# Attention, MoE and gated softmax in one kernel: the 1e-9 of the denominators is summed from memory instead of added

## The chip, the cores and the metric

The kernel runs on one core of a Trainium2 chip. The metric is the device time of one execution in microseconds (us); the kernel before has a median of 773.45 us over three runs. TensorE is called PE (its weight loads PEld), VectorE DVE, ScalarE ACT, GpSimd POOL, and the queue that issues most DMAs SP.

## The reference

Three stages follow each other. Only the first matters here: an attention over keys and values averaged in groups of four rows ("pooled"), plus an attention over the seven keys nearest to each query ("local"). Both softmaxes add 1e-9 to the sum of the exponentials.

```python
def sm_attn(qq, kk, vv):
    s = scale * np.matmul(qq, kk.transpose(0, 1, 3, 2))
    s = s - np.max(s, axis=-1, keepdims=True)
    a = np.exp(s)
    a = a / (np.sum(a, axis=-1, keepdims=True) + 1e-09)
    return np.matmul(a, vv)
# q_d, k_d, v_d: means over factor = 4 rows; batch 4, heads 8, seq 576, head_dim 64
out_d = sm_attn(q_d, k_d, v_d)
out_up = np.repeat(out_d, factor, axis=2)
mask = np.abs(pos[:, None] - pos[None, :]) < factor
# local: scores masked, exp, / (sum + 1e-09), times v
x = out_up + out_local            # to [2304, 512]
x = (x @ w_a) * (x @ w_b) @ w_out # 512 -> 1536 -> 512
# then h = x @ w_in (512 -> 1024), h * softmax(h), layer norm, @ w_out2
```

## The kernel before

The 2304 tokens are handled in six tiles of 384. Every product of the second and third stage is made of three fp32r matmuls (high by high, high by low, low by high; lines 956 to 958), and these fill PE. The attention is done beside them.

**The head.** The first tile's attention runs before the large products. Its pooled part works on four pairs of heads: ACT writes the exponentials of a pair to `p_head` and their sums, by the accumulator of the activation, to `hp_sum` [96, 4, 2] (`head_pooled_exp`, line 1157). DVE makes `hp_den` = (`hp_sum` + 1e-9) * 4 in one tensor_scalar (`head_pooled_norm`, line 1496) and its reciprocal `hp_inv`; the factor 4 is there because `v_d` holds sums of four rows and not means. The turned exponentials are copied from PSUM to `pT_head` by ACT (line 1169). Some matmuls on ones (line 738, `keep_busy`, reading `xup`, which DVE's first instruction fills at line 1688) keep PE occupied.

**Pooled jobs.** Batches 1 to 3 and the rest of batch 0 have their pooled attention in 20 jobs, placed by a hand-written table of (tile, slot) between PE's large products. A job is: scores (PE, line 889), maximum (DVE, 1473), exponential with its sum into `pool_sum` [128, 2] (ACT, 1177), turn (PE, 899), copy to `pT_pool` (ACT, 1186), `pool_den` = (`pool_sum` + 1e-9) * 4 (DVE tensor_scalar, 1479), reciprocal `pool_inv` (DVE, 1482), values (PE, 913), and the output scaled by `pool_inv` (ACT, 1195) and stored.

**Units of the local attention.** For tiles 1 to 5 the local attention is done on DVE, in ten units (two for each tile), each in 18 steps spread over the slots by `local_at`. Seven products q*k and seven reductions (lines 1588 and 1597) give the scores `p_u` [128, 7, 12]. Then come a minimum with the edge mask (1605), the maximum over seven (1606), the subtraction (1607), the exponential on ACT (1215), the sum over seven (1612), the 1e-9 (1613, `u_den`), the reciprocal (1614) and the normalisation (1615). Twenty-odd products with v (1628, 1636, 1642, 1646) and one addition with the pooled part (1652, into `accT`) end the unit. PE turns `accT` (line 924), ACT and DVE split the result into the next tile's `x_hi` (1261) and `x_lo` (1547).

DVE's queue is in program order. Between the steps of the units stand the pooled jobs' steps and those of the large products: `gate` (1554, reads the b product from PSUM), `ab_low` (1558), `wo_low` (1537). POOL runs the low halves of the weights (1900, 1908) and sums of raw rows (1881, 1888) at its own pace, from the point on at which ACT or a DMA has brought their inputs.

Of the kernel before, what the change touches and what calls it, by code (L numbers as in the profile page):

```python
# [5 lines left out]
FP32 = mybir.dt.float32  # L6
FP32R = mybir.dt.float32r
ALU = mybir.AluOpType
ACT = mybir.ActivationFunctionType
# [4 lines left out]
R4 = 4  # L14
# [143 lines left out]
def build_program(nc, q, k, v, w_a, w_b, w_out, w_in, w_out2, g_ln, out):  # L158
# [46 lines left out]
    g_sb = place("g_sb", [128, GC], FP32)  # L205
    p_u = place("p_u", [128, EDGE, HPP * TPP], FP32)
    u_max = place("u_max", [128, HPP * TPP], FP32)
    u_sum = place("u_sum", [128, HPP * TPP], FP32)
    u_den = place("u_den", [128, HPP * TPP], FP32)
    u_inv = place("u_inv", [128, HPP * TPP], FP32)  # L210
    pool_bias = place("pool_bias", [128, 2], FP32)
    pool_sum = place("pool_sum", [128, 2], FP32)
    pool_den = place("pool_den", [128, 2], FP32)
    pool_inv = place("pool_inv", [128, 2, 2], FP32)
    hp_bias = place("hp_bias", [96, PPB, 2], FP32)
    hp_sum = place("hp_sum", [96, PPB, 2], FP32)
    hp_den = place("hp_den", [96, PPB, 2], FP32)
# [141 lines left out]
    with ctx:  # L359
# [757 lines left out]
        def _(act):  # L1117
# [36 lines left out]
            def head_pooled_exp(c):  # L1154
                act.wait_ge(s.hp_bias_ready, c + 1 if c < 2 else PPB)
                for h in range(2):
                    last = A(p_head[:, c, h, :], hp_scores(c, h), ACT.Exp,
                             bias=hp_bias[:, c, h:h + 1], accum_out=hp_sum[:, c, h:h + 1])
                last.then_inc(s.hp_exped, 1)
# [7 lines left out]
            def head_pooled_pT(c):  # L1167
                act.wait_ge(s.hp_turned, c + 1)
                A(pT_head[:, c, :], bank(HP_T[c], 4 * 96, SH), ACT.Copy).then_inc(s.hp_pT_ready, 1)

            def pooled_exp(i):
                at_least(act, s.p_turned, i)
                act.wait_ge(s.pool_bias_ready, i + 1)
                at_least(act, s.pool_inv_ready, i)
                count, _ = job_rows(i)
                for h in range(2):
                    last = A(p_pool[0:count, h, :], bank(XB[h], SD, count), ACT.Exp,
                             bias=pool_bias[0:count, h:h + 1],
                             accum_out=pool_sum[0:count, h:h + 1])
                last.then_inc(s.pool_exped, 1)  # L1180

            def pT_copy(i):
                at_least(act, s.out_mm_d, i)
                act.wait_ge(s.p_turned, i + 1)
                count, _ = job_rows(i)
                A(pT_pool[:, :, 0:count], bank(XB[1])[0:SH].rearrange("p (x e) -> p x e", x=4)[:, :, 0:count], ACT.Copy
                  ).then_inc(s.pT_out, 1)

# [24 lines left out]
            def unit_exp(u):  # L1213
                act.wait_ge(s.u_sub_ready, u - 1)
                A(p_u[:, :, :], p_u[:, :, :], ACT.Exp, scale=SCALE).then_inc(s.u_exped, 1)

# [195 lines left out]
        def _(dve):  # L1412
# [63 lines left out]
            def pooled_inverse(i):  # L1476
                dve.wait_ge(s.pool_exped, i + 1)
                count, _ = job_rows(i)
                chain.link(V.tensor_scalar(pool_den[0:count, :], pool_sum[0:count, :], 1e-9, float(R4),
                                           ALU.add, ALU.mult))  # L1480
                at_least(dve, s.out_d_ready, i - 1)
                V.reciprocal(pool_inv[0:count, i % 2, :], pool_den[0:count, :]).then_inc(s.pool_inv_ready, 1)
# [11 lines left out]
            def head_pooled_norm(c):  # L1494
                dve.wait_ge(s.hp_exped, c + 1)
                chain.link(V.tensor_scalar(hp_den[:, c, :], hp_sum[:, c, :], 1e-9, float(R4), ALU.add, ALU.mult))
                if c >= 2:
# [76 lines left out]
            def local_step(m, g, step, marks, used):  # L1574
# [25 lines left out]
                if step == EDGE + 1:  # L1600
                    local.wait()
                    dve.wait_ge(s.edge_ready, 2)
                    limit = edge[:, m % 3].unsqueeze(2).to_broadcast([128, EDGE, HPP, TPP])
                    by_head = p_u[:, :, :].rearrange("p e (h t) -> p e h t", t=TPP)
                    local.link(V.tensor_tensor(by_head, by_head, limit, ALU.min))
                    local.link(V.tensor_reduce(u_max[:, :], p_u[:, :, :].rearrange("p e n -> p n e"), AX.X, ALU.max))
                    V.tensor_tensor(p_u[:, :, :], p_u[:, :, :],
                                    u_max[:, :].unsqueeze(1).to_broadcast([128, EDGE, HPP * TPP]), ALU.subtract
                                    ).then_inc(s.u_sub_ready, 1)
                if step == EDGE + 2:  # L1610
                    dve.wait_ge(s.u_exped, u - 1)
                    local.link(V.tensor_reduce(u_sum[:, :], p_u[:, :, :].rearrange("p e n -> p n e"), AX.X, ALU.add))
                    local.link(V.tensor_scalar(u_den[:, :], u_sum[:, :], 1e-9, None, ALU.add))
                    local.link(V.reciprocal(u_inv[:, :], u_den[:, :]))
                    V.tensor_tensor(p_u[:, :, :], p_u[:, :, :],
                                    u_inv[:, :].unsqueeze(1).to_broadcast([128, EDGE, HPP * TPP]), ALU.mult
# [70 lines left out]

            V.memset(xup[:, 0:2, :], 1.0).then_inc(s.ones_ready, 1)
            head_qT(0)
            head_kT(0)  # L1690
# [305 lines left out]
```

## Time and profile before

| | us |
|---|---|
| median of 3 runs | 773.45 |
| lowest, highest of the 3 | 771.84, 1066.27 |
| the profiled execution | 773.61 |
| its span in the trace | 771.5 |

| engine | busy us | share of the span |
|---|---|---|
| PE | 759.5 | 98% |
| PEld | 702.9 | 91% |
| DVE | 547.9 | 71% |
| ACT | 301.6 | 39% |
| POOL | 174.6 | 23% |

The three runs agree to about 2 us but for one far above the others. The profiled execution lies 2.1 us above its own span: that much lies around the part which the trace shows. A busy share says how full an engine is over the whole span, and not whether another engine waits for it at a given point: that is read from idle times and what ended them. Times of single instructions are shown in us from the span's start.

### The profile page before, as it was taken

The page shows a single profiled execution, that of the slowest core. Times are in us where ns is not written, and L with a number is a line of the kernel's source. Part 1 is how long each engine was busy: PE and PEld are TensorE (multiplying, and loading weights), DVE is VectorE, ACT ScalarE, POOL GpSimd, SP SyncE. Part 2 cuts the span into 40 slices and gives each one's busy share as a digit, 9 for nine tenths or more (in the row PEclk, how much of TensorE's full clock was granted, in tenths as well). Part 3 has the DMA queues.
Part 4 walks back from the last instruction along what each step waited for, and adds up shares of the span by engine and source line. Part 5 has one row for each costly group of instructions (what it writes and reads, how often), then busy time and mean ns, then how long its engine had stood idle before and what let it go on. Part 6 is the DMA issues. An engine that isn't in the chain of part 4 may idle for free.

```text
span 771.5 us, 12627 instructions
## 1 busy us (share of the span) xinstructions
PE 759.5 (98%) x4616; PEld 702.9 (91%) x4616; DVE 547.9 (71%) x990; ACT 301.6 (39%) x824; POOL 174.6 (23%) x216
## 2 busy tenths in 40 slices
PE   8999999999999999999999999999999999999998
PEld 7889999999999999999999999999988888888886
DVE  5699889989877887797876874023377666666663
ACT  4656446463524434362525343234422222222222
POOL 3349460184444030060001121111100000000000
PEclk9899999999999999999999999999999999999999
DMA  9999947778789575573645523736111111011011
GB/s 179 220 218 228 215 109 219 229 208 237 216 207 257 150 209 153 160 199 114 178 140 165 164 93 103 232 100 202 40 57 56 40 43 55 28 55 55 28 42 41
DMA packets 94650, 108.84 MB, mean 141 GB/s; under 512 B 29309, under 2 KB 62589, under 8 KB 94589
## 3 DMA queue, kind: packets, MB, share of 16 engines
q1 hardware_dynamic: 83293, 99.38, 48.6%
q10 hardware_dynamic: 11296, 8.65, 3.7%
q8 instruction: 37, 0.61, 0.3%
q14 instruction: 24, 0.20, 0.1%
HBM read 87.46 MB, written 20.55 MB: 140 GB/s over the span
## 4 chain that ended last, share of the span: by engine, by line
PE 94%; DVE 2%; SPq 2%; DMA 1%; issue 1%; ACT 0%; DVEq 0%
PE psum L956 28%; PE psum L958 27%; PE psum L957 27%; PE psum L1083 2%; PE psum L913 2%; PE psum L889 1%; PE psum L865 1%; PE psum L924 1%; PE psum L899 1%; DMA v_h<-in_v 1%; SPq L483 1%; SPq L477 1%; SPq L492 1%; PE psum L794 1%; PE psum L738 0%
## 5 line engine op out<-in xcount | busy, mean ns | idle before, releaser
L956 PE MATMUL psum<-x_hi,w_hi 128*128 128x384 f32 x576 | 198.1, 344 | 0.2 <-DVE x_lo L1547 0.2
L958 PE MATMUL psum<-x_hi,w_lo 128*128 128x384 f32 x576 | 193.0, 335 | 0.0
L957 PE MATMUL psum<-x_lo,w_hi 128*128 128x384 f32 x576 | 192.7, 335 | 0.0
L956 PEld LDWEIGHTS psum<-x_hi,w_hi 128*128 128x128 f32 x576 | 108.2, 188 | 3.7 <-issue 2.9
L957 PEld LDWEIGHTS psum<-x_lo,w_hi 128*128 128x128 f32 x576 | 108.3, 188 | 0.0
L958 PEld LDWEIGHTS psum<-x_hi,w_lo 128*128 128x128 f32 x576 | 108.1, 188 | 0.0
L956 PE MATMUL psum<-ab_hi,wo_hi 128*128 128x384 f32 x288 | 99.6, 346 | 0.7 <-DVE wo_lo L1537 0.7
L958 PE MATMUL psum<-ab_hi,wo_lo 128*128 128x384 f32 x288 | 96.5, 335 | 0.0
L957 PE MATMUL psum<-ab_lo,wo_hi 128*128 128x384 f32 x288 | 96.4, 335 | 0.0
L1554 DVE TENSOR_TENSOR ab_f<-psum,a_sb 128x384 f32<-128x384 f32 x72 | 39.9, 554 | 76.9 <-PE psum L958 53.7
L1266 ACT ACTIVATE a_sb<-psum 128x384 f32<-128x384 f32 x72 | 35.3, 490 | 109.9 <-PE psum L958 108.4
L1271 ACT ACTIVATE ab_hi<-ab_f 128x384 fp32r<-128x384 f32 x72 | 37.6, 523 | 93.6 <-DVE ab_f L1554 90.6
L1588 DVE TENSOR_TENSOR tmp<-q_u,k_u 128x768 f32<-128x768 f32 x70 | 71.5, 1025 | 0.0
L1914 POOL TENSOR_TENSOR ab_lo<-ab_f,ab_hi 128x384 fp32r<-128x384 f32 x24 | 28.5, 1188 | 182.7 <-ACT ab_hi L1271 182.7
L1597 DVE TENSOR_REDUCE p_u<-tmp 128x12 f32<-128x768 f32 x70 | 66.0, 942 | 0.1
L1881 POOL TENSOR_TENSOR raw<-raw 96x256 f32<-96x256 f32 x42 | 39.3, 959 | 109.1 <-DMA raw<-in_q 54.6
L1303 ACT ACTIVATE e_sb<-psum,neg_max 128x1024 f32<-128x1024 f32 x18 | 20.1, 1117 | 108.6 <-DVE neg_max L1771 108.6
L956 PE MATMUL psum<-w_hi,lnT_hi 128*128 128x512 f32 x144 | 57.6, 400 | 0.0
L956 PEld LDWEIGHTS psum<-ab_hi,wo_hi 128*128 128x128 f32 x288 | 54.1, 188 | 3.0 <-issue 2.8
L958 PE MATMUL psum<-w_hi,lnT_lo 128*128 128x512 f32 x144 | 56.3, 391 | 0.0
L956 PE MATMUL psum<-win_hi,y_hi 128*128 128x512 f32 x144 | 56.1, 390 | 0.0
L958 PE MATMUL psum<-win_hi,y_lo 128*128 128x512 f32 x144 | 56.1, 389 | 0.0
(163 smaller groups left out, 1364.6 us busy)
## 6 DMA issues: line engine op xcount, KB each, us to landing
wo_hi<-wo_hi_scratch SPq DMA_DIRECT2D x53, 256.0 KB, 2.7
wo_lo<-wo_lo_scratch SPq DMA_DIRECT2D x53, 256.0 KB, 3.0
wo_raw<-in_moe_w_out SPq DMA_DIRECT2D x19, 256.0 KB, 5.6
yT_scratch<-y_sb ACTq DMA_DIRECT2D x6, 768.0 KB, 4.7
y_raw<-yT_scratch SPq DMA_DIRECT2D x18, 256.0 KB, 3.0
out<-out_sb SPq DMA_DIRECT2D x18, 256.0 KB, 2.1
k_u<-in_k SPq DMA_DIRECT2D x11, 384.0 KB
v_u<-in_v SPq DMA_DIRECT2D x11, 384.0 KB
```

What stands on the lines that cost most here:

```text
L913: last = mm(bank(XB[0])[p0:p0 + n, SD + h * D:SD + (h + 1) * D], pT_pool[:, 2 * h + kh, p0:p0 + n], v_d[:, pair, kh, h * D:(h + 1) * D], s ...
L956: mm(dst, wh, xh, start=first, stop=False, skip_group_check=not check)
L957: mm(dst, wh, xl, start=False, stop=False, skip_group_check=not check)
L958: last = mm(dst, wl, xh, start=False, stop=end, skip_group_check=not check)
L1266: A(a_sb[:, g % 2, :], bank(GA, NT), ACT.Copy).then_inc(s.a_copied, 1)
L1271: A(ab_hi[:, g % 2, :], ab_f[:, g % 2, :], ACT.Copy).then_inc(s.ab_hi_ready, 1)
L1303: A(e_sb[:, par, :], psum[:, HB[par][0] * BANK:HB[par][0] * BANK + F2], ACT.Exp, bias=neg_max[:, par:par + 1], accum_out=e_sum[:, par:par ...
L1554: V.tensor_tensor(ab_f[:, g % 2, :], bank(GB, NT), a_sb[:, g % 2, :], ALU.mult).then_inc(s.ab_ready, 1)
L1588: last = V.tensor_tensor(tmp[:, step % 3], q_u[:, :, :], k_u[:, :, step * D:step * D + TPP * D], ALU.mult)
L1597: last = V.tensor_reduce(p_u[:, step - 1, :], tmp[:, (step - 1) % 3] .rearrange("p h (t d) -> p (h t) d", d=D), AX.X, ALU.add)
L1881: last = G.tensor_tensor(t[:, :, i, 0:128], t[:, :, i, 0:128], t[:, :, i, 128:256], ALU.add)
L1914: G.tensor_tensor(ab_lo[:, g % 2, :], ab_f[:, g % 2, :], ab_hi[:, g % 2, :], ALU.subtract).then_inc(s.ab_lo_by_pool, 1)
```

## The change

The constant is no longer added by an instruction. It lies in memory beside the sums, and the sum takes it in:

- `p_u` gets an eighth row, filled with 1e-9 once at the start. The sum of a unit goes over eight rows instead of seven, `u_den` and its instruction are gone, and the reciprocal reads `u_sum`. All other accesses of `p_u` are cut to the first seven rows.
- `pool_sum` and `hp_sum` get a last axis of two. ACT writes the sum to element 0, element 1 holds 1e-9. `pool_den` and `hp_den` are a tensor_reduce over that axis instead of a tensor_scalar.
- The factor 4 that this tensor_scalar also applied goes as 1/4 into the scale of ACT's copies to `pT_head` and `pT_pool`.
- Three memsets on DVE, behind the one of `xup`, write the constants.
- With `u_den` gone and `p_u` larger, what is placed behind them in SBUF (`q_u`, `k_u`, `v_u`, `tmp`, `raw`, `qdT`, `win_hi` and others) lies 64 bytes lower.

```diff
-    p_u = place("p_u", [128, EDGE, HPP * TPP], FP32)
+    p_u = place("p_u", [128, EDGE + 1, HPP * TPP], FP32)
-    u_den = place("u_den", [128, HPP * TPP], FP32)
-    pool_sum = place("pool_sum", [128, 2], FP32)
+    pool_sum = place("pool_sum", [128, 2, 2], FP32)
-    hp_sum = place("hp_sum", [96, PPB, 2], FP32)
+    hp_sum = place("hp_sum", [96, PPB, 2, 2], FP32)
...
-                A(pT_head[:, c, :], bank(HP_T[c], 4 * 96, SH), ACT.Copy).then_inc(s.hp_pT_ready, 1)
+                A(pT_head[:, c, :], bank(HP_T[c], 4 * 96, SH), ACT.Copy, scale=1.0 / R4).then_inc(s.hp_pT_ready, 1)
...
-                             accum_out=pool_sum[0:count, h:h + 1])
+                             accum_out=pool_sum[0:count, h, 0:1])
...
-                A(p_u[:, :, :], p_u[:, :, :], ACT.Exp, scale=SCALE).then_inc(s.u_exped, 1)
+                A(p_u[:, 0:EDGE, :], p_u[:, 0:EDGE, :], ACT.Exp, scale=SCALE).then_inc(s.u_exped, 1)
...
-                chain.link(V.tensor_scalar(pool_den[0:count, :], pool_sum[0:count, :], 1e-9, float(R4),
-                                           ALU.add, ALU.mult))
+                chain.link(V.tensor_reduce(pool_den[0:count, :], pool_sum[0:count, :, :], AX.X, ALU.add))
...
-                chain.link(V.tensor_scalar(hp_den[:, c, :], hp_sum[:, c, :], 1e-9, float(R4), ALU.add, ALU.mult))
+                chain.link(V.tensor_reduce(hp_den[:, c, :], hp_sum[:, c, :, :], AX.X, ALU.add))
...
                     local.link(V.tensor_reduce(u_sum[:, :], p_u[:, :, :].rearrange("p e n -> p n e"), AX.X, ALU.add))
-                    local.link(V.tensor_scalar(u_den[:, :], u_sum[:, :], 1e-9, None, ALU.add))
-                    local.link(V.reciprocal(u_inv[:, :], u_den[:, :]))
-                    V.tensor_tensor(p_u[:, :, :], p_u[:, :, :],
+                    local.link(V.reciprocal(u_inv[:, :], u_sum[:, :]))
+                    V.tensor_tensor(p_u[:, 0:EDGE, :], p_u[:, 0:EDGE, :],
...
             V.memset(xup[:, 0:2, :], 1.0).then_inc(s.ones_ready, 1)
+            V.memset(hp_sum[:, :, :, :], 1e-9)
+            V.memset(pool_sum[:, :, :], 1e-9)
+            V.memset(p_u[:, EDGE, :], 1e-9)
```

No queue is reordered. On DVE, around the third pooled job and the softmax of the second unit (the job's `pool_den` is the first row), the program of before has:

```order
L1479 TENSOR_SCALAR pool_den<-pool_sum 128x2
L1482 RECIPROCAL pool_inv<-pool_den 128x2
L1597 TENSOR_REDUCE p_u<-tmp 128x12
L1537 TENSOR_TENSOR wo_lo<-wo_raw,wo_hi 128x512
L1605 TENSOR_TENSOR p_u<-p_u,edge 128x84
L1606 TENSOR_REDUCE u_max<-p_u 128x12
L1607 TENSOR_TENSOR p_u<-p_u,u_max 128x84
L1612 TENSOR_REDUCE u_sum<-p_u 128x12
L1613 TENSOR_SCALAR u_den<-u_sum 128x12
L1614 RECIPROCAL u_inv<-u_den 128x12
L1615 TENSOR_TENSOR p_u<-p_u,u_inv 128x84
```

The same place in the program of after:

```order
L1478 TENSOR_REDUCE pool_den<-pool_sum 128x2
L1480 RECIPROCAL pool_inv<-pool_den 128x2
L1595 TENSOR_REDUCE p_u<-tmp 128x12
L1535 TENSOR_TENSOR wo_lo<-wo_raw,wo_hi 128x512
L1603 TENSOR_TENSOR p_u<-p_u,edge 128x84
L1604 TENSOR_REDUCE u_max<-p_u 128x12
L1605 TENSOR_TENSOR p_u<-p_u,u_max 128x84
L1610 TENSOR_REDUCE u_sum<-p_u 128x12
L1611 RECIPROCAL u_inv<-u_sum 128x12
L1612 TENSOR_TENSOR p_u<-p_u,u_inv 128x84
```

One row is gone, one has another operation, the order is the same. In all, DVE has ten rows fewer (`u_den`) and three more (the memsets).

## Rows read from the trace of the kernel before

**Rows 1.** The page: busy us (share of the span) xinstructions
```profile
PE 759.5 (98%) x4616; PEld 702.9 (91%) x4616; DVE 547.9 (71%) x990; ACT 301.6 (39%) x824; POOL 174.6 (23%) x216
```

**Rows 2.** Timeline of PE: start us, us, instruction [idle before <-releaser]
```profile
128.48 0.52 PE L924 MATMUL psum<-ident,accT 128*128 128x128 f32 x3 [1.12 <-DVE accT L1652]
...
188.80 0.52 PE L924 MATMUL psum<-ident,accT 128*128 128x128 f32 x3 [0.97 <-DVE accT L1652]
```

**Rows 3.** PE's waits: engine line, waited for: us in total, times, longest
```profile
PE psum L956 <- DVE wo_lo L1537: 0.7, 1, 0.7
PE psum L889 <- DVE x_lo L1547: 0.5, 1, 0.5
```

**Rows 4.** Windows: length; busy us of PE, PEld, DVE, ACT, POOL; clock; DMA, GB/s
```profile
26.00:28.00 2.00, 2.00 (x11) 1.93 (x10) 0.61 (x3) 1.65 (x7) 0.89 (x1) 0.50 1.16 203
99.10:128.40 29.30, 28.25 (x192) 25.80 (x190) 28.53 (x45) 17.30 (x53) 11.85 (x12) 1.00 0.53 148
200.00:771.50 571.50, 567.74 (x3194) 523.20 (x3192) 377.21 (x677) 200.16 (x519) 79.22 (x96) 1.00 0.41 118
```

**Rows 5.** Lines by form: busy us, mean ns of one | idle before, releaser
```profile
L1479 DVE TENSOR_SCALAR pool_den<-pool_sum 96x2 f32<-96x2 f32 x12 | 3.5, 288 | 0.0
L1613 DVE TENSOR_SCALAR u_den<-u_sum 128x12 f32<-128x12 f32 x10 | 2.0, 204 | 0.3
L1150 ACT ACTIVATE qdT<-psum 128x288 f32<-128x288 f32 x6 | 4.1, 760 | 3.3 <-PE psum L865 3.0 <-PE psum L871 0.3
L1150 ACT ACTIVATE kdT<-psum 128x288 f32<-128x288 f32 x6 | 4.0, 740 | 7.4 <-PE psum L865 5.9 <-PE psum L871 0.9 <-ACT y_sb L1276 0.5
```

**Rows 6.** Timeline of DVE, third pooled job and second unit
```profile
109.41 0.70 DVE L1479 TENSOR_SCALAR pool_den<-pool_sum 128x2 f32<-128x2 f32 x1
...
114.01 0.17 DVE L1613 TENSOR_SCALAR u_den<-u_sum 128x12 f32<-128x12 f32 x1
114.22 0.23 DVE L1614 RECIPROCAL u_inv<-u_den 128x12 f32<-128x12 f32 x1
```

**Rows 7.** Single lines of DVE: duration ns min/median/max, first and last start us, forms
```profile
L1479 DVE TENSOR_SCALAR pool_den<-pool_sum x20: 154/158/894, 56.1 to 457.0; 96x2 f32<-96x2 f32 x12, 128x2 f32<-128x2 f32 x8
L1612 DVE TENSOR_REDUCE u_sum<-p_u x10: 286/304/309, 65.9 to 451.3; 128x12 f32<-128x84 f32 x10
L1597 DVE TENSOR_REDUCE p_u<-tmp x70: 934/942/954, 47.7 to 447.5; 128x12 f32<-128x768 f32 x70
L1771 DVE TENSOR_REDUCE neg_max<-part_max x18: 154/155/155, 558.0 to 750.9; 128x1 f32<-128x2 f32 x18
L1615 DVE TENSOR_TENSOR p_u<-p_u,u_inv x10: 245/247/579, 66.9 to 452.1; 128x84 f32<-128x84 f32 x10
```

**Rows 8.** Timeline of POOL, where the first `pool_den` of rows 6 runs
```profile
109.35 0.73 POOL L1900 TENSOR_TENSOR w_lo<-w_raw,w_hi 128x256 fp32r<-128x256 f32 x1 [0.60 <-ACT w_hi L1236]
```

**Rows 9.** Timeline of DVE ahead of the second turn
```profile
156.63 0.31 DVE L1612 TENSOR_REDUCE u_sum<-p_u 128x12 f32<-128x84 f32 x1 [2.71 <-ACT p_u L1215]
...
157.44 0.58 DVE L1615 TENSOR_TENSOR p_u<-p_u,u_inv 128x84 f32<-128x84 f32 x1
...
175.20 2.74 DVE L1588 TENSOR_TENSOR tmp<-q_u,k_u 128x768 f32<-128x768 f32 x1
177.86 0.70 DVE L1479 TENSOR_SCALAR pool_den<-pool_sum 96x2 f32<-96x2 f32 x1
...
178.67 0.93 DVE L1588 TENSOR_TENSOR tmp<-q_u,k_u 128x768 f32<-128x768 f32 x1
```

**Rows 10.** Timeline of POOL in the same stretch
```profile
157.19 0.73 POOL L1908 TENSOR_TENSOR wo_lo<-wo_raw,wo_hi 128x256 fp32r<-128x256 f32 x1 [4.92 <-ACT wo_hi L1250]
...
177.09 1.45 POOL L1908 TENSOR_TENSOR wo_lo<-wo_raw,wo_hi 128x256 fp32r<-128x256 f32 x1
```

**Rows 11.** Timeline of DVE at the start: start us, us, instruction [idle before <-releaser]
```profile
0.86 0.27 DVE L1688 MEMSET xup<- 128x256 f32 x1 [0.86 <-PEq L1986]
5.33 0.46 DVE L1426 COPY qT<-psum 128x288 f32<-128x288 f32 x1 [4.20 <-PE psum L751]
```

More of the change, by code:

```diff
@@ L1157, in head_pooled_exp @@
                     last = A(p_head[:, c, h, :], hp_scores(c, h), ACT.Exp,
-                             bias=hp_bias[:, c, h:h + 1], accum_out=hp_sum[:, c, h:h + 1])
+                             bias=hp_bias[:, c, h:h + 1], accum_out=hp_sum[:, c, h, 0:1])
                 last.then_inc(s.hp_exped, 1)
@@ L1185, in pT_copy @@
                 count, _ = job_rows(i)
-                A(pT_pool[:, :, 0:count], bank(XB[1])[0:SH].rearrange("p (x e) -> p x e", x=4)[:, :, 0:count], ACT.Copy
-                  ).then_inc(s.pT_out, 1)
+                A(pT_pool[:, :, 0:count], bank(XB[1])[0:SH].rearrange("p (x e) -> p x e", x=4)[:, :, 0:count], ACT.Copy,
+                  scale=1.0 / R4).then_inc(s.pT_out, 1)
             def out_d_copy(i):
@@ L1603, in local_step @@
                     limit = edge[:, m % 3].unsqueeze(2).to_broadcast([128, EDGE, HPP, TPP])
-                    by_head = p_u[:, :, :].rearrange("p e (h t) -> p e h t", t=TPP)
+                    by_head = p_u[:, 0:EDGE, :].rearrange("p e (h t) -> p e h t", t=TPP)
                     local.link(V.tensor_tensor(by_head, by_head, limit, ALU.min))
-                    local.link(V.tensor_reduce(u_max[:, :], p_u[:, :, :].rearrange("p e n -> p n e"), AX.X, ALU.max))
-                    V.tensor_tensor(p_u[:, :, :], p_u[:, :, :],
+                    local.link(V.tensor_reduce(u_max[:, :], p_u[:, 0:EDGE, :].rearrange("p e n -> p n e"), AX.X, ALU.max))
+                    V.tensor_tensor(p_u[:, 0:EDGE, :], p_u[:, 0:EDGE, :],
                                     u_max[:, :].unsqueeze(1).to_broadcast([128, EDGE, HPP * TPP]), ALU.subtract
@@ L1612, in local_step @@
                     local.link(V.tensor_reduce(u_sum[:, :], p_u[:, :, :].rearrange("p e n -> p n e"), AX.X, ALU.add))
-                    local.link(V.tensor_scalar(u_den[:, :], u_sum[:, :], 1e-9, None, ALU.add))
-                    local.link(V.reciprocal(u_inv[:, :], u_den[:, :]))
-                    V.tensor_tensor(p_u[:, :, :], p_u[:, :, :],
+                    local.link(V.reciprocal(u_inv[:, :], u_sum[:, :]))
+                    V.tensor_tensor(p_u[:, 0:EDGE, :], p_u[:, 0:EDGE, :],
                                     u_inv[:, :].unsqueeze(1).to_broadcast([128, EDGE, HPP * TPP]), ALU.mult
```

## Prediction

> **What bounds the kernel now.** I read the page's busy shares first: PE is busy 98% of the span, DVE 71% [rows 1]. A change on DVE can then only help where PE waits for DVE. I next took PE's waits by releaser. In the steady part DVE is named as late by two turns of `accT`, 1.12 us ahead of 128.48 and 0.97 ahead of 188.80 [rows 2], and by one product that waits for `wo_lo` (0.7) and one that waits for `x_lo` (0.5) [rows 3]. The windows say where such waits can be: from 200 us to the end PE is busy 567.74 of 571.50 us, and DVE for 377.21 only [rows 4]. So a gain has to come from the first 200 us, where the windows show DVE full (28.53 of 29.30 us between 99 and 128 us) [rows 4].
>
> **What the change takes from DVE.** (1) `u_den`: ten instructions of 204 ns in the mean [rows 5]. On the path the saving is the distance from its start to that of the reciprocal, 114.22 - 114.01 = 0.21 us [rows 6], as the wait on its own result goes too. (2) The sum over eight rows instead of seven: 12 elements more. From 84 to 768 elements the same kind of reduce goes from 304 to 942 ns [rows 7], 0.93 ns an element, so 0.01 us. A unit saves 0.20 us, ten units 2.0. (3) `pool_den`: the mean of twelve of the twenty is 288 ns [rows 5], but the median of all only 158 and the longest 894 [rows 7]. I take 0.29 us for each. The long ones are waits: that at 109.41 lasts 0.70 us to 110.11, and a POOL instruction beside it runs 109.35 to 110.08 [rows 8]; that at 177.86 ends at 178.56, and a POOL instruction ends at 178.54 [rows 9, 10]. The tensor_reduce with two outputs of two elements each isn't in the trace. From below its price is bounded by the reduce of two elements to one, 155 ns, from above by 304 ns for 84 elements [rows 7]; it is much nearer to the first, and I take 0.16. The question is whether it waits for POOL. The 70 reduces of line 1597 stay within 934 to 954 ns and the ten sums within 286 to 309 [rows 7], through stretches in which POOL works. So I take no wait, and twenty jobs save 20 * (0.29 - 0.16) = 2.6 us of DVE. The other end is that it waits as the tensor_scalar did and nothing is saved. (4) `hp_den` is the same operation on two elements, four times, in the head; at the same price 4 * (0.29 - 0.16) = 0.5 us. PE's waits for DVE in the head don't come from it (its first turns of `p_head` stand behind other products), so none of this is put on the path. Sum: 5.1 us, 1% of DVE's busy time.
>
> The Trainium skill, page SBUF — State Buffer, section Who interferes with whom, has a rule for (3): tensor_scalar can take the port pair that DVE shares with GpSimd and then one blocks the other for a whole instruction, while a tensor_reduce on trn2 never contends. By it `pool_den` costs 0.16 us in every job; if it didn't hold, the main term below would fall from 0.54 to zero. The durations of lines 1597 and 1612 agree with it.
>
> **What it adds.** Three memsets of 4 to 16 elements. DVE's own of 256 elements took 0.27 us [rows 11], and a smaller one can't cost more, so they are between 0 and 0.8 us together. They stand behind the one that PE waits for, and DVE then idles 4.20 us until PE's first turns are done [rows 11]. They cost nothing; without that cover they would cost up to 0.8 us. The scale of 1/4 in ACT's copies: the copy to `qdT` has a scale and takes 760 ns, that to `kdT` has 1.0 and takes 740 [rows 5], the same within the spread, on an engine that is 39% busy [rows 1]: nothing. At most it is 24 * 0.02 = 0.5 us of ACT. The 64 bytes by which buffers move, the strided accumulator write and the seven-row views: no row prices them; they change no count of elements, and I take zero, with the range's ends for the rest.
>
> **What of it reaches PE.** DVE's head start is lost wherever DVE itself waits for PE or ACT. The stretches that end in a turn are therefore cut at the last such wait.
>
> First turn (128.48). DVE last waited long at 99 us; from there it is busy 28.53 of 29.30 us [rows 4]. In between lie one long `pool_den` at 109.41 (0.70 becomes 0.16, 0.54 saved), followed on the queue by a reciprocal and a reduce of line 1597, one `u_den` (0.20 saved), and one `pool_den` that was short. 0.54 + 0.20 = 0.74 us, against a wait of 1.12 [rows 2]. I take 0.74. The bounds are 0 (the reduce waits for POOL as well, or a two-input instruction behind it loses what it saved, and the next one the rest) and 1.12.
>
> Second turn (188.80). DVE last waited at 156.63, 2.71 us for ACT [rows 9]. The `u_den` behind it saves 0.20, but line 1615, two instructions on, took 0.58 us [rows 9] instead of its median of 0.25 [rows 7], because it ran into a POOL instruction of 157.19 to 157.92 [rows 10]. Coming 0.20 earlier it meets the same one and ends at the same time: nothing. The `pool_den` at 177.86 loses its 0.54, but the product at 178.67 has two inputs and now meets the POOL instruction that ends at 178.54. It can start 0.13 earlier and not 0.54. And the product at 175.20 lasted 2.74 us, the same product at 178.67 0.93 [rows 9]: it stood behind POOL, so what was saved ahead of it is lost too. I take 0.13, with bounds 0 and 0.97, the whole wait [rows 2].
>
> The wait for `x_lo` (0.5 us) stands behind the second turn; what DVE gains there has moved PE as well, so it is not shortened a second time. The wait for `wo_lo` (0.7) I leave as it is, since DVE idles for PE between the first unit's softmax and that instruction and gives up there what it has saved, and I keep its whole for the low end [rows 3]. Behind 200 us DVE has room [rows 4], and I expect nothing there.
>
> **Sum.** 0.74 + 0.13 = 0.87 us. Against the profiled execution's 773.61 us (its span and 2.1 us around it) this is 772.7 us. That execution stands 0.16 us above the median, so the forecast is about 0.1% under either. A difference of under 2%, some 15.5 us, can't be told from no change here, and this one is far below it.
>
> **Rivals.**
> - *Nothing arrives* (0.17). All that DVE saves is taken by its next wait for POOL, as at 157.44, also ahead of the first turn: 773.3 to 773.9 us. For it speaks that line 1615 does just this [rows 9]; against it that a reduce of 0.94 us, which doesn't wait for POOL [rows 7], follows the long `pool_den` of the first stretch.
> - *The order at the lock turns round* (0.11), on the other side. A DVE instruction that now starts just ahead of a row of POOL instructions starts just behind one. The product at 175.20 paid 2.74 - 0.93 = 1.8 us so [rows 9], and PE's slack there is used up, so it costs PE about the same: 773.6 - 0.9 + 1.8 = 774.5, with two such places 776.3. It decides from 0.9 us on, where it eats the gain. Against: the savings move DVE by 0.2 to 0.7 us only, about as often to the better.
> - *All waits for DVE go* (0.05): 773.6 - 1.1 - 1.0 - 0.7 - 0.5 = 770.3 us.
> - *The head's clock* (0.07). Between 26 and 28 us PE's granted clock is 0.50, its 1.2 GHz level [rows 4]; this window gives 1 us of full-speed work for 2 us. If the dip were gone, the time would be at least 1 us less, and with two such windows more of it 2 us more: 771.7 or less, or 774.7. The change touches nothing ahead of it except the memsets.
> - *More than 2% either way* (0.02). For that PE would have to stand for 15 us; no row shows a mechanism.
> - *The forecast*: 0.58, with a range of its own of 771.9 to 773.4.
>
> **Chances and range.** Within 2%: 0.98, and 0.01 on each side. The range runs from the case in which all waits go, or the dip does, to one reversal at the lock and part of a second one: 770.0 to 775.5 us.
>
> **What would show it.** `pool_den` as a reduce within 150 to 200 ns in all twenty jobs, longest included (if one takes 0.7 us beside POOL, the reading of the lock is wrong). `u_sum` at about 315 ns. The wait before the first turn at about 0.4 us instead of 1.12, that before the second at 0.8 or more. DVE's busy time down by about 5 us. The three memsets ended before 3 us and PE's first turns unmoved. PE's waits by DVE over 3.3 us in sum, or a DVE product of over 2 us at a new place, would show that the order at the lock has changed and would make the prediction too low.

## The result, and the profile after

The changed kernel takes 775.1 us (median of 22 runs) against 771.53 us of the kernel before (22 runs, taken beside them). The ratio is 1.0043, with a 95% interval of 1.0029 to 1.0058; it is taken over the fast executions, without two of the kernel before at 1066 and 4274 us. The change makes the kernel slower by 0.4%, 2.2 to 4.5 us (3.3 by the ratio; the medians differ by 3.6). That is inside the range of the prediction and too small for the 2% bound, but it is on the other side of zero than the forecast, and the interval leaves no doubt about the sign.

The profiled execution of the changed kernel has 774.66 us, a span of 772.9 us and a mean clock of 0.996, the same clock as that of before (span 771.5). These two can be laid beside each other. The page, busy us (share of the span) xinstructions:

```profile
PE 762.4 (99%) x4616; PEld 702.8 (91%) x4616; DVE 543.5 (70%) x983; ACT 301.5 (39%) x824; POOL 173.7 (22%) x216
```

DVE has 4.4 us less than in [rows 1], as it should. But PE, with the same 4616 instructions, is busy for 2.9 us more, and PE is the engine that fills the span. The first question is therefore why the same matmuls take longer, and only the second what became of the waits.

**The waits** did what they were meant to do. PE's waits in the changed kernel (engine line, waited for: us in total, times, longest):

```profile
PE psum L898 <- ACT p_pool L1176: 1.2, 2, 0.9
PE psum L923 <- DVE accT L1649: 0.6, 2, 0.3
PE psum L888 <- DVE x_lo L1545: 0.4, 1, 0.4
```

Those for `accT` come to 0.6 us instead of 2.09 [rows 2], the one for `wo_lo` [rows 3] is gone, and the longer one for `p_pool`, of 0.9, is new. The same on PE's timeline (start us, us, instruction [idle before <-releaser]); the last row is the turn of the fifth tile:

```profile
126.46 0.52 PE L923 MATMUL psum<-ident,accT 128*128 128x128 f32 x3 [0.31 <-DVE accT L1649]
...
175.15 0.53 PE L898 MATMUL psum<-ident,p_pool 96*72 96x96 f32 x4 [0.86 <-ACT p_pool L1176]
...
187.07 0.52 PE L923 MATMUL psum<-ident,accT 128*128 128x128 f32 x3 [0.25 <-DVE accT L1649]
...
369.51 0.33 PE L923 MATMUL psum<-ident,accT 128*128 128x128 f32 x1 [0.62 <-ACT out_d L1194]
```

The kernel before reaches that turn later:

```profile
371.11 0.33 PE L924 MATMUL psum<-ident,accT 128*128 128x128 f32 x1 [0.62 <-ACT out_d L1195]
```

So at 370 us the changed kernel is 1.60 us ahead. Five places account for 1.37 of it: 0.81 and 0.72 less at the two turns, the 0.67 for `wo_lo` gone, 0.03 less for `x_lo`, 0.86 more for `p_pool`. How much of this lead is due to the change is another question. The wait for `wo_lo` comes and goes by itself (below), and single executions of kernels with the same instructions spread more: from the first product on `x` to the first on `win` it is 511.99 us in the kernel before and 510.43 in the changed one, but 511.0 to 514.0 over the eight kernels of this study that have the instructions of before, and 512.2 to 512.8 in the three others that have those of the changed kernel.

**The loss** comes behind that point, where I had expected nothing. The third stage opens with the products of `win` and `y`. The first of them in the kernel before:

```profile
551.60 0.39 PE L956 MATMUL psum<-win_hi,y_hi 128*128 128x512 f32 x1
```

and in the changed kernel:

```profile
549.95 0.39 PE L955 MATMUL psum<-win_hi,y_hi 128*128 128x512 f32 x1
```

From there to the end of the span it is 771.5 - 551.60 = 219.90 us before and 772.9 - 549.95 = 222.95 after: 3.05 us more. (The span is given to 0.1 us, so such a length is good to 0.05.) With the lead of 1.65 us this makes the 1.4 us by which the spans differ. PE doesn't wait longer in this stretch. From 200 us on it is idle 3.79 us against 3.76 in [rows 4], and in the third stage alone 3.17 against 3.14. The second row is the third stage of the kernel before, the third that of the changed kernel (length; busy us of PE, PEld, DVE, ACT, POOL; clock; DMA, GB/s):

```profile
200.00:772.90 572.90, 569.11 (x3182) 521.42 (x3180) 375.32 (x671) 199.60 (x516) 76.72 (x90) 1.00 0.41 116
...
551.60:771.50 219.90, 216.76 (x1033) 181.03 (x1032) 141.50 (x321) 53.73 (x95) 10.88 (x19) 1.00 0.14 45
...
549.95:772.90 222.95, 219.78 (x1033) 180.78 (x1032) 141.76 (x321) 53.77 (x95) 10.92 (x19) 1.00 0.14 44
```

The lines by form (line, operation, tile, shape xcount | busy us, mean ns of one) say which matmuls are longer. Before:

```profile
L956 PE MATMUL psum<-x_hi,w_hi 128*128 128x384 f32 x576 | 198.1, 344 | 0.2 <-DVE x_lo L1547 0.2
...
L956 PE MATMUL psum<-win_hi,y_hi 128*128 128x512 f32 x144 | 56.1, 390 | 0.0
L958 PE MATMUL psum<-win_hi,y_lo 128*128 128x512 f32 x144 | 56.1, 389 | 0.0
L957 PE MATMUL psum<-w_lo,lnT_hi 128*128 128x512 f32 x144 | 56.1, 389 | 0.0
L957 PE MATMUL psum<-win_lo,y_hi 128*128 128x512 f32 x144 | 56.1, 389 | 0.0
```

After:

```profile
L955 PE MATMUL psum<-x_hi,w_hi 128*128 128x384 f32 x576 | 198.1, 344 | 0.2 <-DVE x_lo L1545 0.2
...
L955 PE MATMUL psum<-win_hi,y_hi 128*128 128x512 f32 x144 | 56.8, 395 | 0.0
L957 PE MATMUL psum<-win_hi,y_lo 128*128 128x512 f32 x144 | 56.8, 394 | 0.0
L956 PE MATMUL psum<-win_lo,y_hi 128*128 128x512 f32 x144 | 56.8, 394 | 0.0
...
L956 PE MATMUL psum<-w_lo,lnT_hi 128*128 128x512 f32 x144 | 56.3, 391 | 0.0
```

The products of 384 columns are the same. The 432 products on `win` (512 columns each) are 5 ns longer each. These matmuls overlap, so the distance from one start to the next says more than the duration. Two neighbouring `win_hi,y_hi` products, three products apart, stand in the kernel before at

```profile
603.03 0.39 PE L956 MATMUL psum<-win_hi,y_hi 128*128 128x512 f32 x1
603.26 0.39 PE L957 MATMUL psum<-win_lo,y_hi 128*128 128x512 f32 x1
603.48 0.39 PE L958 MATMUL psum<-win_hi,y_lo 128*128 128x512 f32 x1
603.71 0.39 PE L956 MATMUL psum<-win_hi,y_hi 128*128 128x512 f32 x1
```

and in the changed one at

```profile
602.09 0.39 PE L955 MATMUL psum<-win_hi,y_hi 128*128 128x512 f32 x1
602.33 0.39 PE L956 MATMUL psum<-win_lo,y_hi 128*128 128x512 f32 x1
602.56 0.39 PE L957 MATMUL psum<-win_hi,y_lo 128*128 128x512 f32 x1
602.79 0.39 PE L955 MATMUL psum<-win_hi,y_hi 128*128 128x512 f32 x1
```

0.68 us became 0.70. Over the last fifteen of the eighteen token tiles of this stage the mean distance is 226.8 ns before and 233.3 ns after; 432 * 6.5 ns = 2.8 us, nearly the whole 3.05. (In the first three tiles it is 4.6 ns, which makes it 2.7.)

### The profile page after: what moved, and what is told of

Read it like the earlier page. It is cut to its first block, busy times and chain, and to the rows that moved or that the text cites. A ratio compares the mean times of both kernels' runs of the same rounds, so it can differ in the third digit from the quotient of the medians.

```text
span 772.9 us, 12620 instructions
## 1 busy us (share of the span) xinstructions
PE 762.4 (99%) x4616; PEld 702.8 (91%) x4616; DVE 543.5 (70%) x983; ACT 301.5 (39%) x824; POOL 173.7 (22%) x216
## 4 chain that ended last, share of the span: by engine, by line
PE 93%; DVE 2%; SPq 2%; issue 1%; ACT 1%; DMA 1%; DVEq 0%
PE psum L955 28%; PE psum L957 27%; PE psum L956 27%; PE psum L1082 2%; PE psum L912 2%; PE psum L888 1%; PE psum L864 1%; PE psum L898 1%; PE psum L923 1%; SPq L482 1%; SPq L491 1%; SPq L476 1%; DMA v_h<-in_v 1%; PE psum L793 1%; PE psum L737 0%
## 5 line engine op out<-in xcount | busy, mean ns | idle before, releaser
L956 PE MATMUL psum<-win_lo,y_hi 128*128 128x512 f32 x144 | 56.8, 394 | 0.0
## 6 DMA issues: line engine op xcount, KB each, us to landing
yT_scratch<-y_sb ACTq DMA_DIRECT2D x6, 768.0 KB, 5.3
```

Of the source, the lines that this page charges most:

```text
L956: mm(dst, wh, xl, start=False, stop=False, skip_group_check=not check)
```

## The experiments

The instructions of the third stage are the same in both kernels, and the granted clock is 1.00 in both. What differs is where its buffers lie. Without `u_den` every buffer placed behind it starts 64 bytes lower (sizes are rounded up to 64 bytes, so the larger `p_u`, `pool_sum` and `hp_sum` move nothing), `win_hi` and `win_lo` among them (in a partition, `win_hi` starts at byte 163200 before and 163136 after); `y_hi` and `y_lo`, which lie over `x_hi` and `x_lo`, are placed ahead of it and stay (bytes 127104 and 139392). In these products `win` is the moving operand, with 512 columns, and `y` is the one that is loaded as the weights. My theory was that the 64 bytes cost the 3 us and the rest of the change gains about what was forecast. The rival was that the addresses don't matter, and the loss comes from the change's other parts.

**The 64 bytes put back** into the changed kernel, so that all buffers lie as before:

```diff
+    at["next"] += 64
     u_inv = place("u_inv", [128, HPP * TPP], FP32)
```

> The changed kernel with 64 unused bytes put in front of u_inv, so that q_u, k_u, tmp, raw, qdT, win_hi, win_lo and all else lie where they lay before; nothing else differs from it. Theory A (the address): the 432 matmuls that read win_hi or win_lo as their moving operand start every 0.2335 us in the changed kernel and every 0.2267 us before; this comes from the 64 bytes, so here they are back at 0.2267 us (mean 389 ns), 2.9 us are returned, and the time is 771 to 772.5 us, level with before or up to 1 us under it. Theory B (the new operations themselves: reduces, scales, timing at the lock between VectorE and GpSimd): the matmuls stay at 394 ns and the time stays at 774 to 775. If both hold in part, the matmuls are fast and the time is still over that of before: then what is left is B's part.

**The 64 bytes alone**, in the kernel before (`hp_bias` uses the unused end of `pool_bias`'s place, and all that follows moves down by 64):

```diff
-    hp_bias = place("hp_bias", [96, PPB, 2], FP32)
+    hp_bias = place("hp_bias", [96, PPB, 2], FP32, at["next"] - 224)
```

> The kernel before, with hp_bias laid into the unused half of pool_bias's 64 bytes; everything from hp_sum on, among it q_u, k_u, tmp, raw, qdT, win_hi and win_lo, lies 64 bytes lower, as in the changed kernel. No instruction differs. Theory A: the matmuls on win_hi and win_lo take 394 ns in the mean instead of 389 and start every 0.2335 us; the time is 2.9 us over before, 774.4. Theory B: no change, 771.5.

With the bytes back, the changed kernel takes 770.63 us (12 runs; before 771.71), ratio 0.9989 (0.9966 to 1.0012), and its stage 3 takes 219.92 us from the first product on `win`. The kernel before with the shift alone takes 775.58 us, ratio 1.0048 (1.0029 to 1.0068), and 222.92 us for the stage. It has no instruction of the change in it. Its lines by form are those of the changed kernel to the nanosecond:

```profile
L956 PE MATMUL psum<-win_hi,y_hi 128*128 128x512 f32 x144 | 56.8, 395 | 0.0
L958 PE MATMUL psum<-win_hi,y_lo 128*128 128x512 f32 x144 | 56.8, 394 | 0.0
L957 PE MATMUL psum<-win_lo,y_hi 128*128 128x512 f32 x144 | 56.8, 394 | 0.0
```

The rival is refuted: the 3 us go with the address, with or without the rest of the change.

**`win` alone moved**, in the kernel before, by 64 and by 128 bytes. Is it that `win` must start at some multiple of bytes (it started at 128 behind a multiple of 256), or something else?

```diff
-    win_hi = place("win_hi", [128, F2C], FP32R, att_at)
-    win_lo = place("win_lo", [128, F2C], FP32R, att_at + 4 * F2C)
-    win_raw = place("win_raw", [128, F2C], FP32, att_at + 4 * F2C)
+    win_hi = place("win_hi", [128, F2C], FP32R, att_at + 64)
+    win_lo = place("win_lo", [128, F2C], FP32R, att_at + 4 * F2C + 64)
+    win_raw = place("win_raw", [128, F2C], FP32, att_at + 4 * F2C + 64)
```

> The kernel before with only win_hi, win_lo and win_raw 64 bytes higher; q_u, tmp, raw and the rest stay where they were. Theory A in its narrow form (only the start of the moving operand counts): the same 2.9 us as with all buffers moved, 774.4. A second form (other buffers' addresses, read by VectorE or written by DMAs, cost something as well): less than with all moved. Theory B: 771.5.

> The kernel before with win_hi, win_lo and win_raw 128 bytes higher. If it is the offset within 128 bytes that counts, the matmuls stay at 389 ns and 0.2267 us apart. If any move away from the old place costs (a clash with another buffer), they are slow. If 256 bytes count, they are faster or slower than 389, since the old start is an odd multiple of 128.

With 64 the kernel takes 773.1 us, ratio 1.0016 (1.0000 to 1.0032), and the stage 221.64 us. With 128, a place that is again a multiple of 128, one execution takes 772.3 us, and the stage takes 222.86 us, as slow as the changed kernel. The 64 bytes cost half of what the narrow form of my theory asked (1.4 us in the time and 1.7 in the stage, for 2.9). The first of the three lines by form with 128:

```profile
L956 PE MATMUL psum<-win_hi,y_hi 128*128 128x512 f32 x144 | 56.9, 395 | 0.0
```

So "a start at a multiple of 128 bytes is fast" is refuted. What was left were a period of 256 bytes in the place of `win` itself, or in its distance from `y`. The times of single executions can't tell 3 us apart here. The head's clock isn't the reason, since it was 1.00 in all of those below; the first two stages take different times from one execution to the next. The third stage began at 547.34 us with `win` + 128 and at 550.05 with `win` + 256, with the same instructions. The length of the stage and the distance of the starts can tell, and they are what I went by.

**`win` moved by 256 bytes** in the kernel before (as above, 256 for 64):

> The kernel before with win_hi, win_lo and win_raw 256 bytes higher, so that the start is the same within 256 bytes. In the kernel before a product on win starts 544 TensorE cycles (0.2267 us) after the last, in the changed kernel 560; 64 bytes higher it was 550, 128 bytes higher 558. If what counts is the start within 256 bytes: 544 again. If it is the distance to another buffer or a longer period: any other value up to 560.

**Only `win` put back** in the changed kernel (as above, + 64; everything else stays 64 lower):

> The changed kernel with only win_hi, win_lo and win_raw put back to their old place, 64 bytes higher; all the other buffers stay 64 bytes lower than before. If the place of win alone decides: 544 cycles from product to product and the whole 2.9 us of the third stage back. If the place of another buffer takes part: it stays near 560.

Both are fast, 219.85 and 219.91 us for the stage (772.05 and 772.38 us, with 772.12 for the kernel before beside them). The second one says that of all buffers that moved, `win` alone carries the loss.

**`x` and `y` moved by 64, all behind them by 128**, in the kernel before. If only the place of `win` counted, this would be as slow as 128 above (222.9 us); if the distance counts, it should be as 64 above (221.6):

```diff
+    at["next"] += 64
     x_at = at["next"]
...
+    at["next"] += 64
     a_sb = place("a_sb", [128, 2, NT], FP32)
```

> The kernel before with x_hi, x_lo and what shares their place (y_hi, y_lo) 64 bytes higher, a_sb to ident and all behind 128 bytes higher. x_hi and x_lo are the moving operands of 1,728 matmuls of 384 columns, 416 cycles apart before. If a start 64 bytes off a multiple of 128 slows every moving operand, they go to some 430 cycles: 1,728 * 16 / 2400 = 11 us more, 783. If it is special to the third stage's products, they stay at 416; win moves by 128 bytes and y by 64, and the third stage tells how the distance of the two counts.

**`win` moved by 192**, a distance of 64 below the next multiple of 256:

> The kernel before with win 192 bytes higher, which is the place of the changed kernel plus 256. If the start within 256 bytes decides: 560 cycles, as in the changed kernel.

The first gives 221.03 us for the stage and 772.07 in all, on the side of the distance. It also refutes that any start off a multiple of 128 bytes costs every product, which asked for 16 cycles (7 ns) more for each of the 1728 products on `x_hi` and `x_lo`, now off it by 64: they start every 173.4 ns, against 173.8 before. Their distance from their weights `w` went from 0 to 64 bytes as well, so a distance of 64 doesn't cost these products of 384 columns anything. The products on `ab`, whose distance from `wo` went from 0 to 128, went from 174.0 to 175.6 ns. The second gives 222.91 us, as the changed kernel with the same distance.

**`y` moved by 192** in the changed kernel, `win` left where the change put it. If the distance counts, this must be fast, and it is the opposite operand that is moved:

```diff
-    y_hi = place("y_hi", [128, 2, DC, 128], FP32R, x_at)
-    y_lo = place("y_lo", [128, 2, DC, 128], FP32R, x_lo_at)
-    y_raw = place("y_raw", [128, 2, DC, 128], FP32, x_lo_at)
+    y_hi = place("y_hi", [128, 2, DC, 128], FP32R, x_at + 192)
+    y_lo = place("y_lo", [128, 2, DC, 128], FP32R, x_lo_at + 192)
+    y_raw = place("y_raw", [128, 2, DC, 128], FP32, x_lo_at + 192)
```

> The changed kernel; only y_hi, y_lo and y_raw, the stationary operands of the products on win, lie 192 bytes higher inside the space of x_hi and x_lo, so that they start at 64 within 256 bytes, as win does there. win isn't moved. If the distance of the two operands within 256 bytes decides, it is 0 again: 544 cycles and 219.9 us from the first product on win to the end of the span, 3.0 us less than the changed kernel's 222.9, and a time of 771 to 772. If the moving operand's own place decides: 560 cycles and 775.

```profile
L955 PE MATMUL psum<-win_hi,y_hi 128*128 128x512 f32 x144 | 56.1, 390 | 0.0
L956 PE MATMUL psum<-win_lo,y_hi 128*128 128x512 f32 x144 | 56.1, 390 | 0.0
L957 PE MATMUL psum<-win_hi,y_lo 128*128 128x512 f32 x144 | 56.1, 389 | 0.0
```

The products are back at 390 ns, the stage takes 220.68 us, and the kernel 771.42 us (before 771.68), ratio 0.9997 (0.9978 to 1.0016). So for these products the distance decides, and not the place of either operand: `win` at 64 behind a multiple of 256 is slow with `y` at 128 and fast with `y` at 64.

**The two halves of the change apart**, with the buffers where they were. The pooled half (the axis of two in `pool_sum` and `hp_sum`, the tensor_reduce, the scale of 1/4, two memsets), and the unit's half (eight rows in `p_u`, no `u_den` instruction but its place kept, one memset):

```diff
-                chain.link(V.tensor_scalar(pool_den[0:count, :], pool_sum[0:count, :], 1e-9, float(R4),
-                                           ALU.add, ALU.mult))
+                chain.link(V.tensor_reduce(pool_den[0:count, :], pool_sum[0:count, :, :], AX.X, ALU.add))
```

> The kernel before with the pooled part of the change alone (pool_den and hp_den as a tensor_reduce over two, 1/4 in the copies' scale, two memsets); no address moves. pool_den within 140 to 155 ns in all jobs. Of the gain ahead of the first turn 0.54 of 0.74 us should be here: about 0.5 us under before, 771.1, and no more than 1.1 us. If the timing at the lock eats it: the same as before.

```diff
-                    local.link(V.tensor_scalar(u_den[:, :], u_sum[:, :], 1e-9, None, ALU.add))
-                    local.link(V.reciprocal(u_inv[:, :], u_den[:, :]))
+                    local.link(V.reciprocal(u_inv[:, :], u_sum[:, :]))
```

> The kernel before with the unit part alone (eighth row of p_u, no u_den instruction, one memset); u_den's 64 bytes are kept, so no address moves. The sum at 320 ns, 0.2 us saved in a unit: 0.2 us under before by the first turn, about 771.4, which this comparison can hardly tell from no change. If the new operations were the cause of the slower time: over before in one of this and the pooled part.

The pooled half takes 771.5 us, ratio 1.0003 (0.9982 to 1.0023); the unit's half 770.28 us, ratio 0.9976 (0.9955 to 0.9997), against 771.68 before. I had expected 771.1 and 771.4. The intervals overlap each other and that of the whole change with its bytes put back, so by time alone it isn't settled which half brings a gain. The waits say more, because they repeat. PE's wait ahead of the first turn is 1.09 to 1.16 us in the eight kernels with the instructions of before, 0.96 with the unit's half, 0.54 with the pooled half, and 0.31 to 0.34 in the four kernels with the whole change. So the pooled half gives 0.6 us there and the unit's half 0.2, as the prediction split it (0.54 and 0.20). PE's waits with the pooled half:

```profile
PE psum L899 <- ACT p_pool L1177: 1.1, 2, 0.8
...
PE psum L924 <- DVE accT L1651: 0.8, 2, 0.5
```

With the unit's half:

```profile
PE psum L924 <- DVE accT L1651: 1.9, 2, 1.0
...
PE psum L899 <- ACT p_pool L1177: 0.6, 1, 0.6
```

The unit's half is the only kernel of this study whose interval lies below 1, and it keeps a reduction of work that the trace shows (ten instructions fewer on DVE, one memset more). It is the version I would keep, but its gain is small: part of the 0.2% is the head's clock (below), which was under full speed in one of its twelve executions and in nine of the 29 of before. Among those at full clock the medians are 770.25 and 770.99 us, 0.1% apart.

**`win` moved by 32**, to see whether the cost grows with the distance:

> The kernel before with win 32 bytes higher. Steps so far: distance 0 gives 544 cycles, +64 gives 550, +128 gives 558, -64 gives 560. If the cost rises with the distance: between 544 and 550, by about 2 us less than at -64. If any start off a multiple of 64 costs extra: 560 or more.

It doesn't: 32 bytes are as slow as 128 or 192 (774.26 us in one execution; the stage took 223.17 us). But this is also the only kernel in which an operand starts off a multiple of 64 bytes, and nothing here separates the two. All together, with the mean from one start to the next of the products on `win`, worked out from the last fifteen tiles of each timeline:

| kernel | distance of `win` from `y`, modulo 256 bytes | start to start, ns | stage 3, us |
|---|---|---|---|
| before | 0 | 226.8 | 219.90 |
| after, 64 bytes put back | 0 | 226.8 | 219.92 |
| pooled half | 0 | 226.8 | 219.95 |
| unit's half | 0 | 226.8 | 219.87 |
| before, `win` + 256 | 0 | 226.8 | 219.85 |
| after, `win` + 64 | 0 | 226.8 | 219.91 |
| after, `y` + 192 | 0 | 227.3 | 220.68 |
| before, `win` + 32 | 32 | 233.4 | 223.17 |
| before, `win` + 64 | 64 | 229.3 | 221.64 |
| before, `x`, `y` + 64, `win` + 128 | 64 | 229.0 | 221.03 |
| before, `win` + 128 | 128 | 232.7 | 222.86 |
| after | 192 | 233.3 | 222.95 |
| before, all behind `u_den` - 64 | 192 | 233.3 | 222.92 |
| before, `win` + 192 | 192 | 233.3 | 222.91 |

Seven kernels at distance 0 are within 0.5 ns, and the seven others are 2.2 to 6.6 ns above the first of them. The length at one distance repeats to 0.5 ns, at 0 and at 64 whichever operand was moved. Why 64 costs less than 32 isn't explained by anything here.

## Why the prediction was wrong, point by point

**The step that failed** is the one on "the 64 bytes by which buffers move", which I put together with the strided write and the seven-row views and priced at zero, because "they change no count of elements". It cost 3.05 us, in the third stage, of which I had written that I "expect nothing there". The prediction looked at this stage for waits only, and the cost is no wait: it lies in the time of each matmul. Equal counts of elements were no reason for a zero, since these 432 matmuls have the same counts before and after and start 6.5 ns further apart. What it should have said is: `win` is the operand of 432 matmuls on the engine that fills the span, its place changes and that of `y` doesn't, and no row prices that. At 2 ns for each, such a term already eats the gain of 0.87 us. That the measured 775.1 us lies inside the stated range, and near the 774.5 of one rival, is luck: the range's upper end was made of reversals at the lock, and the 3.05 us have nothing to do with the lock.

**The start of the sum** was too high as well. It was 773.61 us, the profiled execution, which has the clock dip in its head (below); the median of 22 executions of the kernel before is 771.53.

**DVE's savings** were sized well. Single lines of the changed kernel (duration ns min/median/max, first and last start us, forms), for [rows 7]:

```profile
L1478 DVE TENSOR_REDUCE pool_den<-pool_sum x20: 138/144/151, 56.0 to 455.3; 96x2 f32<-96x4 f32 x12, 128x2 f32<-128x4 f32 x8
L1610 DVE TENSOR_REDUCE u_sum<-p_u x10: 312/320/327, 65.1 to 449.6; 128x12 f32<-128x96 f32 x10
```

No `pool_den` takes over 151 ns, where one took 894. I had forecast 150 to 200 ns, so it is even below the price I took, and the twenty together fell from 5.8 to 2.9 us, by 2.9 for the forecast 2.6. The Trainium skill, page SBUF — State Buffer, section Who interferes with whom, has a tensor_reduce on trn2 never contend for the port pair that DVE shares with GpSimd. The trace agrees: all twenty are short, where the tensor_scalar was held up beside POOL's work. The sum over eight rows takes 320 ns for 304, 0.016 us where 0.01 was forecast. DVE's busy time fell by 4.4 us for "about 5".

**What was priced at nothing for its cover** was right. The three memsets ran in the head, and DVE still idled 4.24 us before its first copy (4.20 in [rows 11]):

```profile
1.08 0.07 DVE L1686 MEMSET hp_sum<- 96x16 f32 x1
1.13 0.06 DVE L1687 MEMSET pool_sum<- 128x4 f32 x1
1.14 0.07 DVE L1688 MEMSET p_u<- 128x12 f32 x1
...
5.45 0.46 DVE L1425 COPY qT<-psum 128x288 f32<-128x288 f32 x1 [4.24 <-PE psum L750]
```

ACT's busy time is 301.5 us for 301.6, so the scale of 1/4 costs nothing.

**The first turn** lost 0.81 of its 1.12 us; the forecast was 0.74. This repeats in all four kernels with the whole change. With the bytes put back, 0.34 us are left:

```profile
125.63 0.52 PE L924 MATMUL psum<-ident,accT 128*128 128x128 f32 x3 [0.34 <-DVE accT L1650]
```

**The second turn** lost 0.72 us, where I had taken 0.13. But ahead of it stands the new wait of 0.86 us, so the stretch between the two turns had 0.97 us of PE's waits before and has 1.11 now. By the starts it went from 188.80 - 128.48 = 60.32 us [rows 2] to 187.07 - 126.46 = 60.61: 0.29 us lost where 0.13 was to be gained. This repeats too. The five kernels with the pooled half take 60.54 to 60.62 us from turn to turn. The unit's half (60.30) and six of the eight with the instructions of before (60.08 to 60.32) take less, and in the other two PE waited 0.7 us for a `wo_lo` from POOL there. My reading had the stretch keep its order against POOL, and it didn't. **The order at the lock turned round**, the rival on the other side, once, ahead of this turn. Before, the long product stood at 175.20 [rows 9]; after, DVE's timeline has:

```profile
170.61 2.74 DVE L1639 TENSOR_TENSOR acc<-acc,tmp 128x768 f32<-128x768 f32 x1
173.27 0.54 DVE L1552 TENSOR_TENSOR ab_f<-psum,a_sb 128x384 f32<-128x384 f32 x1
173.74 0.44 DVE L1472 TENSOR_REDUCE pool_bias<-psum 96x2 f32<-96x288 f32 x1
```

and POOL's beside it:

```profile
169.95 1.89 POOL L1888 TENSOR_TENSOR raw<-raw 96x128 f32<-96x128 f32 x3
...
171.80 0.73 POOL L1908 TENSOR_TENSOR wo_lo<-wo_raw,wo_hi 128x256 fp32r<-128x256 f32 x1
172.50 1.45 POOL L1908 TENSOR_TENSOR wo_lo<-wo_raw,wo_hi 128x256 fp32r<-128x256 f32 x1
```

The product lasts 2.74 us and ends at 173.35. POOL's fourth instruction ends at 172.53, and what is left from there, 0.82 us, is about the 0.93 that a product of this size took at 178.67 [rows 9]: I read this as the product standing behind four of them. The read of PSUM and the maximum `pool_bias` behind it are late by that, the job's exponential needs that maximum, and PE waits for `p_pool` at 175.15, in the timeline shown above. The rival had this mechanism and asked 1.8 us for it; it came, but in the place of the old long product and not on top of it, so PE paid 0.86 there and got 0.72 back at the turn. It isn't a chance event of one execution. All five kernels with the pooled half have this wait, of 0.81 to 0.86 us, and none of the nine others has it; with the bytes put back it is:

```profile
174.30 0.52 PE L899 MATMUL psum<-ident,p_pool 96*72 96x96 f32 x4 [0.84 <-ACT p_pool L1177]
```

**The wait for `wo_lo`**, which I left as it was, is gone in the changed kernel and is back (0.8 us) with the bytes put back. It isn't tied to the change: it is missing in three of the eight kernels with the instructions of before as well, and 1.4 us long in the changed kernel with `y` + 192.

**The sum of the rest** is smaller than forecast by the waits that repeat: about 0.8 us gained at the first turn and 0.3 lost up to the second, 0.5 us where the prediction had 0.87. The time doesn't contradict either: with the addresses held, the change gives a ratio of 0.9989, 0.85 us, and the interval reaches from 2.6 us faster to 0.9 us slower, so that no gain is shown and the nearness to 0.87 is luck. The term on the first turn was right in mechanism and size, that on the second had the wrong sign, and the missing term gave the sign of the whole. The timed difference, 3.3 us, is larger than 3.05 - 0.85 = 2.2 or 3.05 - 0.5 = 2.5; its interval (2.2 to 4.5) reaches both, and whether something else stands behind the other 1 us stays open.

**The head's clock** differs between executions of one kernel: the clock of 0.50 at 26 to 28 us [rows 4] shows in the profiled executions with a mean clock of 0.995 to 0.996 (before, after, and before with the 64 bytes alone), and in those at 1.00 it doesn't. The dip is longer than the window that the prediction read: in the kernel before the clock is 0.58, 0.50, 0.50 and 0.71 in the four windows of 2 us from 22 us on, which is 3.4 us of full-speed work lost and not 1. The times say the same. Of the 29 executions of the kernel before that were timed beside the two halves, the 20 at full clock have a median of 770.99 us and the nine below it 774.26. The first product on `x` starts at 39.5 to 40.0 us with the dip and at 35.7 to 38.3 without: the pooled half's profiled run has a span of 768.0 us mainly for this reason, with the same stage 3 as before. An equal clock is not enough to lay two single executions beside each other for 1 us, since the stretch from there to the third stage spreads by 3 us (above). What repeats to a few tenths is the third stage, the wait at the first turn and, but for two executions, the stretch between the turns.

## What to carry to other kernels

When an edit takes a buffer away or changes its size, list which operands of the bounding engine's matmuls move relative to each other, and treat that as a term with an unknown price for each matmul, or keep the layout fixed with a pad so that the edit is all that changes. When a kernel is slower with less work on it, compare the mean time of the same instruction before and after (lines by form) before looking for waits: a few ns in each of some hundred matmuls don't show as idle time anywhere.

## What the runs showed of the hardware

- The back-to-back fp32r matmuls on `win` and `y` (512 columns) start every 226.8 to 227.3 ns when the moving operand and the weights start at the same byte modulo 256, and every 229.0 to 233.4 ns at the other distances tried (32, 64, 128, 192). Bringing the distance back to 0, by moving either operand, gives the time back. The mechanism behind it wasn't found. It is no rule for every matmul: the products of 384 columns on `x` and `w` went from 173.8 to 173.4 ns when their distance went from 0 to 64, and those on `ab` and `wo` from 174.0 to 175.6 when it went to 128.
- The stage's other 432 products, on `w2` and `lnT`, whose places are the same in all these kernels, vary as well: `w_lo,lnT_hi` is at 389 ns before and 391 after. Part of it is a trail of the products on `win`. Where a group of `lnT` products follows `win` without a break, in sixteen tiles, the kernel before has 226 to 227 ns from one start to the next at once, and the changed kernel has, in all but the first, about 226, 236, 228, 233 and 231 before it comes to 227: 20 ns for each tile, 0.3 us in all, about the rest of the 3.05 us. With `y` + 192 the three forms are at 402, 393 and 389 ns against 400, 391 and 389 before, which is 0.6 of the 0.8 us by which that kernel's stage is longer. There too the longer distances stand close behind a change of operands. Why they do is open.
- By the traces, a two-input instruction on DVE can stand behind several of POOL's in a row, and not one alone: 2.74 us for one that takes 0.93, behind four of them of which the last ends at 172.53. POOL's next, beside the product, then takes 1.45 us where the one ahead of it took 0.73. The Trainium skill, page SBUF — State Buffer, section Who interferes with whom, has a DVE instruction with two SBUF inputs contend with a GpSimd instruction that reads SBUF, and the one that issues first hold the shared port pair for the whole instruction; the trace has DVE wait for more than one.
- Prices on DVE that the trace of before didn't have: a tensor_reduce from four elements to two takes 144 ns (median of twenty), a memset of 4 to 16 elements 60 to 70 ns.
